# Gathered rows that change partition quarters through memory, with one gather a tile, in the expert stage of an attention and expert-layer kernel

## The reference, cut to what matters

```
logits = x @ w_gate
expert_idx = np.argmax(logits, axis=1)
gate_w = softmax(logits)[np.arange(N), expert_idx]
for e in range(E):
    mask = expert_idx == e
    h = np.maximum(x[mask] @ w1[e], 0.0)
    out[mask] = gate_w[mask, None] * (h @ w2[e])
```

## Time and profile before

| what | value |
|---|---|
| time, median of 3 runs | 1517.04 us (1516.64 to 1517.5) |
| time of the profiled execution | 1513.94 us |
| its span, first to last instruction | 1512.2 us |
| TensorE busy | 1466.0 us |
| VectorE / ScalarE / GpSimd busy | 913.9 / 633.1 / 616.8 us |
| mean granted TensorE clock | 0.989 of full speed |
| attention and first layer | to about 1008 us |
| expert stage | from there to the end |

### The profile page before, as it was taken

The page is one execution under the profiler, slowest core; times in us unless marked ns, Lnnn a source line. Parts: engine busy times, 40 slices in busy tenths (PEclk is TensorE's granted clock), DMA queues, the critical chain, the costliest instruction groups (busy, mean ns, idle before and its releaser), DMA issues.

```text
span 1512.2 us, 29278 instructions
## 1 busy us (share of the span) xinstructions
PE 1466.0 (97%) x7918; PEld 1264.5 (84%) x7919; DVE 913.9 (60%) x1669; ACT 633.1 (42%) x1291; POOL 616.8 (41%) x725
## 2 busy tenths in 40 slices
PE   7999999999999999999999999989899999999997
PEld 6999999999978888888888888877687778778885
DVE  4688888888825374655637465535466656665442
ACT  5688788788812223122222312223243434333221
POOL 5666676676710022020202202110554456666551
PEclk9999999999999999999999999999899999999999
DMA  7354444344430202020120202144677777764441
GB/s 253 114 140 103 108 107 106 102 108 127 107 122 0 70 15 83 0 83 28 56 69 14 83 0 83 15 137 140 191 215 224 232 219 225 226 209 152 143 144 51
DMA packets 113738, 174.05 MB, mean 115 GB/s; under 512 B 54960, under 2 KB 74672, under 8 KB 109474
## 3 DMA queue, kind: packets, MB, share of 16 engines
q1 hardware_dynamic: 104386, 153.39, 34.1%
q0 software_dynamic: 9312, 20.15, 4.3%
HBM read 123.64 MB, written 50.32 MB: 115 GB/s over the span
## 4 chain that ended last, share of the span: by engine, by line
PE 49%; DMA 11%; SPq 4%; issue 4%; POOL 2%; DVE 1%; ACT 1%; POOLq 0%; DVEq 0%; ACTq 0%
PE bank L173 48%; DMA h_scratch<-arena 5%; DMA arena<-we 2%; SPq L1019 1%; DMA rows_scratch<-arena 1%; POOL arena L1103 1%; DMA out<-arena,ids 1%; DMA arena<-rows_scratch,idgq 1%; SPq L830 1%; SPq L1039 1%; SPq L996 0%; DVE xturn L1478 0%; ACT arena L1228 0%; POOLq L830 0%; ACT big L816 0%
## 5 line engine op out<-in xcount | busy, mean ns | idle before, releaser
L173 PE MATMUL bank<-big,xs 128*128 (+1 forms) x2100 | 492.9, 395 | 22.0 <-DVE xs L1483 8.9
L173 PEld LDWEIGHTS bank<-big,xs 128*128 128x128 f32 x2100 | 398.4, 191 | 111.6 <-issue 29.2
L173 PE MATMUL bank<-xs,big 128*128 128x512 f32 x1728 | 397.5, 391 | 2.7 <-PEq L222 2.7
L173 PEld LDWEIGHTS bank<-xs,big 128*128 128x128 f32 x1728 | 324.7, 188 | 70.4 <-issue 3.0
L173 PE MATMUL bank<-big 128*128 128x512 f32 (+1 forms) x1632 | 328.4, 350 | 2.0 <-POOL big L312 1.4
L173 PEld LDWEIGHTS bank<-big 128*128 128x128 f32 (+1 forms) x1632 | 257.8, 166 | 36.7 <-POOL big L312 1.6
L1055 POOL TENSOR_TENSOR arena<-arena 128x512 f32<-128x512 f32 x32 | 46.8, 1473 | 433.3 <-DMA arena<-rec_scratch 433.3
L1440 DVE TENSOR_TENSOR arena<-arena,bank 128x512 f32<-128x512 f32 x72 | 49.4, 687 | 245.9 <-PE bank L173 245.9
L1103 POOL DMA_INDIRECT arena<-rows_scratch,idgq x144 | 146.2, 1015 | 65.9 <-issue 35.5
L1365 DVE CUSTOM_DVE_ANT_0 arena<-arena 128x512 f32<-128x512 f32 x256 | 159.3, 687 | 17.8 <-ACT arena L1220 17.8
L1198 ACT COPY arena<-bank 128x512 f32<-128x512 f32 x72 | 42.4, 589 | 287.9 <-PE bank L173 287.9
(11 more groups left out here) (186 smaller groups left out, 1351.0 us busy)
## 6 DMA issues: line engine op xcount, KB each, us to landing
arena<-we SPq DMA_DIRECT2D x32, 1024.0 KB, 6.0
h_scratch<-arena SPq DMA_DIRECT2D x37, 512.0 KB
arena<-h_scratch SPq DMA_DIRECT2D x148, 128.0 KB
kqraw<-kq SPq DMA_DIRECT2D x32, 576.0 KB, 3.8
xT_scratch<-arena SPq DMA_DIRECT2D x32, 288.0 KB
rows_scratch<-arena SPq DMA_DIRECT2D x36, 256.0 KB, 2.2
arena<-v SPq DMA_DIRECT2D x64, 128.0 KB, 2.4
arena<-xT_scratch SPq DMA_DIRECT2D x8, 1024.0 KB, 5.5
```

What stands on the lines that cost most here:

```text
L173: ins = nc.tensor.matmul(out, left[a], right[b], start=first and n == 0, stop=last and n == 2)
```

## The change

- One gather a tile of whole rows (`gather_far`), for tile g + 3 in place of g + 2. It waits until the rows before it in `xg` have been stored (`x_stored`), not until they have been transposed.
- SP stores `xg` to a scratch of 256 KB (`store_gathered`) and loads it back with quarters exchanged into a new buffer `xq` by four loads of 64 KB (`load_row_quarters`), once the store has landed and `turn_rows` has read `xq`. `turn_rows` reads `xq`.
- In the loop SP's order becomes: store and loads of tile g + 2's rows, store of tile g's hidden rows, weights, loads of the hidden rows. The semaphore `way_open` is only counted up, between waits.
- `idq`, its 16 loads, ScalarE's scaling and the list of quarters are gone. One more table entry is made on VectorE.
- In stage 2 the wait for the row stores, with the freeing of x2, moves from the end of a turn into the next one: ahead of the x loads, and in the last turn behind the loads of weights 0 and 1.
- Chunk 4 of the weights is loaded inside the last turn, ahead of its row stores, and chunk 5 ahead of the wait for these stores. Before, both came behind that wait.

```diff
@@ -131,7 +131,7 @@
-                        ("idq", NQ * E * TPE, F32), ("quarter", 1, U32), ("idgq", NQ, U32),
+                        ("cden", H * S // DK, F32), ("idfar", 1, U32), ("xq", DM, F32),

@@ -139,10 +139,8 @@
-    m["cden"] = m["idq"][:, 0:H * S // DK]
-    m["idf"] = arena[:, SLOTS * CW + 2 * FF:SLOTS * CW + 2 * FF + E * TPE].bitcast(U32)

@@ -158,6 +156,7 @@
+    m["xrows"] = nc.dram_tensor("x_scratch", [P, DM], F32).ap()

@@ -597,8 +596,6 @@
-            for a in range(NQ):
-                dve.memset(m["quarter"][a * (P // NQ):(a + 1) * (P // NQ), :], a)

@@ -852,7 +849,7 @@
-        idf_set, idq_in, xq_in = sem("s3_idf_set"), sem("s3_idq_in"), sem("s3_xq_in")
+        x_stored, xq_in, way_open = sem("s3_x_stored"), sem("s3_xq_in"), sem("s3_way_open")

@@ -956,8 +953,22 @@
             def load_weights(c):
                 sp.dma_start(m["stage"][:, (c % 2) * CW:(c % 2 + 1) * CW], t["we"][c]).then_inc(w_in[c % 2], 16)
+            def load(c):
+                slot = (c % SLOTS) * CW if isinstance(c, int) else sp.snap((c % SLOTS) * CW)
+                sp.wait_ge(w_here, 16 * c)
+                sp.dma_start(ahead[:, ds(slot, CW)], t["we"][ds(c, 1)].rearrange("a p n -> p (a n)")
+                             ).then_inc(w_here, 16)
+
+            def rows_landed(i):
+                if has_before(i):
+                    sp.wait_ge(rows_out, 16 * BQ * i)
+                    sp.sem_inc(x2_free, 1)
+
+            sp.sem_inc(w_here, 16 * CPE)
+
             def turn(i, more):
                 if more:
+                    rows_landed(i)
                     sp.wait_ge(x_lo, DC * i + DC)
                     load_x(sp, m, i + 1)
                     for c in range(DC):
@@ -971,17 +982,18 @@
                     load_weights(0)
                     load_weights(1)
+                    rows_landed(i)
                     for c in range(2, CPE):
                         sp.wait_ge(w_lo, c - 1)
                         load_weights(c)
+                    sp.wait_ge(lg_mm, BQ)
+                    sp.wait_ge(ab_lo, FC * NB)
+                    load(CPE)
                 for q in range(BQ):
                     sp.wait_ge(x2_gated, BQ * i + q + 1)
                     sp.dma_start(m["rows"][ds(i * BT + q * P, P), :], x2[:, q]).then_inc(rows_out, 16)
                 if not has_before(i):
                     sp.wait_ge(m["rec_out"], 16 * B + 16)
-                if more:
-                    sp.wait_ge(rows_out, 16 * BQ * i + 16 * BQ)
-                    sp.sem_inc(x2_free, 1)
             for u in range(2):
                 sp.wait_ge(m["nd_out"][u], 32 * PAIRS // 2)
@@ -990,12 +1002,6 @@
             load_den(sp, m, B - 1)
             turns(sp, turn)
-            def load(c):
-                slot = (c % SLOTS) * CW if isinstance(c, int) else sp.snap((c % SLOTS) * CW)
-                sp.wait_ge(w_here, 16 * c)
-                sp.dma_start(ahead[:, ds(slot, CW)], t["we"][ds(c, 1)].rearrange("a p n -> p (a n)")
-                             ).then_inc(w_here, 16)
-
             def load_into_slot_of(c):
                 sp.wait_ge(w_lo, c + 1)
                 load(c + SLOTS)
@@ -1019,32 +1025,53 @@
                     sp.dma_start(hq[a * Q:(a + 1) * Q, :].rearrange("i (b c) -> i b c", b=P // Q), stored[a]
                                  ).then_inc(hq_in, 16)
+            def store_gathered(g):
+
+                sp.wait_ge(gathered, 16 * g + 16)
+                sp.sem_inc(way_open, 1)
+                sp.wait_ge(xq_in, 16 * NQ * g)
+                sp.sem_inc(way_open, 1)
+                sp.dma_start(m["xrows"], xg).then_inc(x_stored, 16)
+
+            def load_row_quarters(g):
+
+                sp.wait_ge(x_stored, 16 * g + 16)
+                sp.sem_inc(way_open, 1)
+                sp.wait_ge(x_turned, g)
+                sp.sem_inc(way_open, 1)
+                stored = m["xrows"].rearrange("(b i) (a n) -> a i b n", i=Q, a=NQ)
+                for a in range(NQ):
+                    sp.dma_start(m["xq"][a * Q:(a + 1) * Q, :].rearrange("i (b n) -> i b n", b=P // Q), stored[a]
+                                 ).then_inc(xq_in, 16)
+
             def tile(g):
+                store_gathered(g + 2)
+                load_row_quarters(g + 2)
                 store_rows(g, hs)
+                loads_of(g - 1)
                 load_quarters(g)
-                loads_of(g - 1)
-
-            sp.sem_inc(w_here, 16 * CPE)
+
             sp.sem_inc(h_stored, 32)
             sp.sem_inc(hq_in, 128)
-            sp.wait_ge(lg_mm, BQ)
-            sp.wait_ge(ab_lo, FC * NB)
+            sp.sem_inc(x_stored, 16 * (FIRST + 1))
+            sp.sem_inc(xq_in, 16 * NQ * (FIRST + 1))
+            load(CPE + 1)
             sp.wait_ge(rows_out, 16 * BQ * NB)
-            for c in range(CPE, CPE + 3):
-                load(c)
-            sp.wait_ge(idf_set, 1)
-            idq = m["idq"][:].bitcast(U32).rearrange("p (b n) -> p b n", b=NQ)
-            for a in range(NQ):
-                for b in range(NQ):
-                    sp.dma_start(idq[a * Q:(a + 1) * Q, b], m["idf"][b * Q:(b + 1) * Q, :]).then_inc(idq_in, 16)
+            load(CPE + 2)
             sp.wait_ge(w_lo, CPE)
             sp.wait_ge(idt_mm, 1)
             sp.wait_ge(tabs, 2)
+            store_gathered(FIRST + 1)
             store_rows(2, hq)
+            load_row_quarters(FIRST + 1)
             load_quarters(2)
             load(CPE + 3)
-            tiles(sp, tile)
-            loads_of(last_of(sp, 1))
+            tiles(sp, tile, 2)
+            last1 = last_of(sp, 1)
+            store_rows(last1, hs)
+            load_quarters(last1)
+            loads_of(last_of(sp, 2))
+            loads_of(last1)
         @block.gpsimd
         def _(pool):
@@ -1087,24 +1114,18 @@
                 pool.indirect_dma_start(xg, None, m["rows"], bass.IndirectOffsetOnAxis(m["idg"][:, 0:1], 0)
                                         ).then_inc(gathered, 16)
-            def gather_quarters(g):
-
-                row = table(m, pool, ROW, g, 0, E * TPE - 1)
+            def gather_far(g):
+
+                row = table(m, pool, ROW, g, 0, E * TPE)
                 if isinstance(g, int):
-                    pool.wait_ge(xtr_mm, g)
-                else:
-                    pool.wait_ge(x_turned, g)
+                    pool.wait_ge(xtr_mm, FIRST + 1)
+                pool.wait_ge(x_stored, 16 * g)
                 pool.sem_inc(turn_taken, 1)
-                pool.tensor_tensor(m["idgq"][:], idq[:, :, ds(row, 1)].rearrange("p b n -> p (b n)"),
-                                   m["quarter"][:, 0:1].to_broadcast([P, NQ]), ALU.add).then_inc(idg_set, 1)
+                pool.tensor_copy(m["idfar"][:], m["idall"][:, ds(row, 1)]).then_inc(idg_set, 1)
                 pool.wait_ge(idg_set, g + 1)
                 pool.sem_inc(turn_taken, 1)
-                for b in range(NQ):
-                    pool.indirect_dma_start(xg[:, b * P:(b + 1) * P], None,
-                                            m["rows"].rearrange("r (a n) -> (r a) n", a=NQ),
-                                            bass.IndirectOffsetOnAxis(m["idgq"][:, b:b + 1], 0)).then_inc(xq_in, 16)
-
-            idq = m["idq"][:].bitcast(U32).rearrange("p (b n) -> p b n", b=NQ)
+                pool.indirect_dma_start(xg, None, m["rows"],
+                                        bass.IndirectOffsetOnAxis(m["idfar"][:, 0:1], 0)).then_inc(gathered, 16)
             def scatter(g):
                 pool.wait_ge(scattered, 16 * g)
@@ -1145,18 +1166,19 @@
             pool.sem_inc(idg_set, FIRST)
             gather(FIRST)
-            pool.wait_ge(idq_in, 16 * NQ * NQ)
-            gather_quarters(FIRST + 1)
+            gather_far(FIRST + 1)
             pool.wait_ge(y_sb, 2)
             pool.indirect_dma_start(t["out"], bass.IndirectOffsetOnAxis(m["ids0"][:, 0:1], 0), ysb, None,
                                     bounds_check=N - 1, oob_is_err=False).then_inc(scattered, 16)
+            gather_far(FIRST + 2)
             pool.wait_ge(tabs, 2)
             def period(g):
-                gather_quarters(g + 2)
+                gather_far(g + 3)
                 scatter(g - 2)
-            last = tiles(pool, period, 2)
+            last = tiles(pool, period, 3)
+            scatter(last_of(pool, 4))
             scatter(last_of(pool, 3))
             scatter(last_of(pool, 2))
             row = table(m, pool, ROW, last, 0, E * TPE)
@@ -1310,8 +1332,6 @@
             relu(1)
             rows_high(2)
-            act.wait_ge(idt_sb, 1)
-            act.mul(m["idf"], last_ps[:, 0:E * TPE], float(NQ)).then_inc(idf_set, 1)
             weights(CPE)
             relu_stored(2)
@@ -1473,10 +1493,10 @@
             def turn_rows(g):
-                dve.wait_ge(xq_in, 16 * NQ * g - 16 * NQ * FIRST)
+                dve.wait_ge(xq_in, 16 * NQ * g + 16 * NQ)
                 dve.wait_ge(h_mm, 2 * g)
                 dve.transpose(m["xturn"].rearrange("p (c b j) -> p c b j", c=DC, b=P // Q),
```

(3 more changed lines are left out.)

## The result

The changed kernel takes 1577.11 us (median of 4 runs) where the kernel before takes 1516.84 on the same chip: a ratio of 1.039 (1.037 to 1.042), 60 us slower. The forecast was slower too, but by 11 us, and its range ended at 1547. The profiled execution of the changed kernel took 1578.93 us, against 1513.94 before: 65 us between the two traces.

A forecast was written before the change was run, and what follows sets the result against it. TensorE, busy 97% of the span, was taken as the bound, SP's queue next. Gains ahead of the loop would be eaten by 12.6 us turns: second product 25 begins 11.5 us later, 1513.94 becomes 1525.4, median 1528 us; range 1497 to 1547.

The forecast's parts named there:

- x2's gap: Before x2's transposes, ahead of the loop: earlier weights 0 and 1 remove 4.9 us of gap and 3.4 of clock, 8.3 us.
- the prediction's own sign: Ahead of the loop: if TensorE's gap at 1003 stays, the step that removes it by earlier weights fails.
- the rival that named this: Ahead of the loop: moved waits do nothing, row stores and id scatters still hold weights; up to 8 us more, chance 0.05.
- Gather 3's gap: Before gather 3's transposes, ahead of the loop: gather 3 meets an idle queue, 2.3 + 1.7 = 4.0 us go.
- Start of the loop: Tile 4: gather 4 issued at about 1048.4, its hidden rows' store at 1084.3 where it stands near 1091 before.
- The turn: SP's loop turn with a weight load: 12.6 us a tile (12.2 to 13.5), against TensorE's 10.9 and 11.67 before.
- hidden store to weights: SP's loop turn: 0.39 us of issue and 1.94 us of table loads and branches, 2.33 us.
- weights' issue to the store's landing: SP's loop turn: weights, hidden rows and gathered rows' store pass one queue in order; 7.6 us (7.2 to 8.5).
- landing to hidden store: SP's loop turn: 0.3 us of waits, 2.1 for four row loads, 0.25 to the store, 2.65 us.
- Transfers do not hold each other: Loop: gathered rows' store takes its lone 2.2 us even behind weights, turn 10.4; 1490.6 us, or 1482; chance 0.12.
- The queue packs better: Loop: each DMA engine passes on after its own share of weights, 6.5 us for 7.6, turn 11.5; 1504 us; chance 0.18.
- The gather is late: Loop: SP waits for gather g+2, held on POOL behind a scatter waiting for y_sb; about 1550 us; chance 0.08.

The follow-up runs named there:

- 5: The changed kernel with weights 0 and 1 issued ahead of the second-last turn's row stores and id scatters; 1563.3 us, ratio 1.037 to the kernel before.
- 9: The kernel before with the change's stage 2 edits, and weights 0 and 1 issued ahead of the row stores and id scatters; 1499.2 us, ratio 0.993.
- 1: The changed kernel with the gathered rows' store issued a turn earlier, ahead of the weights; 1547.6 us, ratio 1.025 to the kernel before.
- 2: The changed kernel with the weights issued behind the loads of hidden rows; 1615.4 us, ratio 1.070 to the kernel before.
- The stage-2 part alone: The kernel before with only the moved row-store wait and the early loads of weights 4 and 5, loop untouched; 1504.7 us, ratio 0.997.
- 16: The changed kernel with the loop's 24 weight loads cut to their first eighth, all issues, waits and table reads kept; 1505.6 us, ratio 0.996.
- after: The changed kernel itself, against the kernel before; 1577.1 us, ratio 1.039.
- 7: The changed kernel with the gathered rows' store ahead of the weights and two scratch slots for those rows; 1532.0 us, ratio 1.016 to the kernel before.
- 10: The changed kernel with the early gathered store, two scratch slots, and hidden quarters' loads ahead of the weights; 1530.3 us, ratio 1.013 to the kernel before.
- 14: The changed kernel with the loop's weight loads issued by ScalarE on its own queue; 1583.9 us, ratio 1.050 to the kernel before.

## Why the prediction was right in direction and wrong in size

**Ahead of the loop, x2's gap: the step that failed outright.** It said the weights, issued earlier, would land by 997 to 998 behind the row stores. They landed at 1002.2 and 1005.2, 25 and 27 us after issue. The row stores and GpSimd's scatters of ids were issued in the same microseconds; in the trace the row stores landed at 997.1, the last scatter at 1002.4. The weights' packets ran from 987.5 to 1004.9 beside them and took 849 ns each on average, where the kernel before shows 371 for the same packets sent later. The gap at 1003 stayed (7.0 us and its stretch at half clock): by the prediction's own sign the first step fails. It bounded the landing by the earlier trace rows alone. Runs 5 and 9 show what was missing, a place ahead of the stores: there the gap is gone. The price of the rival that named this (up to 8 us) was right; its 0.05 was not.

**Gather 3's gap** went, as said, in every trace with the change or its stage-2 part. In runs 1 and 2 one of 1.8 and 0.6 us came instead ahead of the transposes of an earlier gather (`ids`, tiles 0 to 2). The stage-2 part alone gave 5 us where 8.3 + 4.0 were counted on; run 9, with the first gap gone, gave 0.7%, 11 us.

**Start of the loop.** Tile 4's hidden store was forecast at 1084.3 and came at 1096.65: 12.4 us late. Its gather was issued at 1056.7 instead of 1048.4, x2's 8.3 us not having gone, and took 5 us beside a scatter; the store was issued at 1061.89.

**The turn.** Forecast 12.6 (12.2 to 13.5), measured 14.3. From tile 4's hidden store to tile 25's it took 302.7 us (1096.65 to 1399.37) instead of 267.5: 35.2 us over 21 turns, the largest term. With the 12.4 above that is the 47.6 us by which tile 25's store missed its forecast of 1351.8; behind it the changed kernel took 177.8 us to its end where the forecast has 171.9. By the turn's three steps:
- hidden store to weights: 2.33 forecast, 3.22 measured. In the records of SyncE's instructions the second of the two table reads took 1.15 us instead of 0.27. In each such turn it lies beside the packets of GpSimd's gather; the two reads of 0.27 that the forecast was read off had the hidden rows' 1 KB pieces beside them. Run 16 has the same 3.1, so the weights' packets aren't its cause; that the gather's are is not shown.
- weights' issue to the store's landing: 7.6 forecast, 8.7 measured, above the high end of 8.5. The form of the sum was right (run 16: take the packets away and 2.9 of it goes). By the DMA records (medians of the turns with one load) the weights' last packet ends 4.9 us after their issue, as forecast, and the gathered store's 0.8 behind the hidden rows', as forecast. The hidden rows' last one ends 2.4 behind the weights', not 1.5 to 1.6: that term was read off the store of these 512 KB, and what stands there is their load in 512 pieces of 1 KB. And from the store's last packet to the row loads pass another 0.6, for which the sum had no term.
- landing to hidden store: 2.65 forecast, 2.4 measured.

So the loop's mechanism was right, and the terms of its sum that failed are the first step (0.9 us a turn too small), the load of the hidden rows (0.9) and the unpriced 0.6. Against them stand 0.4, by which the 7.6 lies above the low end, and the 0.3 of the last step: 1.7 us a turn in all.

Turns without weights measured 11.0, not 10.1 to 10.4: no longer covered by 10.9.

**The rivals.** "Transfers do not hold each other" (0.12) is refuted by 16 against after: 2.4 us alone, 5.3 behind weights. The 2.6 us estimate that stands with it is near the lone store's 2.1 and far from the 4.6 to 5.9 of the turns with weights. The fit in the Trainium skill ("DMA: Bandwidth & Descriptors", anatomy of one DMA) that it is worked out from is one for DMAs issued by GpSimd, and this store is issued by SyncE. "The queue packs better" (0.18) is refuted by the 8.7. "The gather is late" is refuted by SyncE's single wait at L1030. All three of the faster and even cases rested on a turn of 12.2 us or less, and the largest doubt was on the other side: every term was read from the kernel before, where the pieces it priced had not yet run beside each other.

**What stays open.** Why the gap before x2's transposes varies from 2.1 to 7.0 us with the same order of issues; why the table read is slow in the changed kernel; and whether larger pieces for the quarter loads would shorten the turn, which wasn't tried. Runs 1, 2, 7, 10 and 14 together bear out that the ring is held by whatever follows the weights on the DMA engines; the landing of each single transfer under another's packets is read from their times, and was not isolated one by one.

## What to carry to other kernels

A bulk load is free only as long as nobody in a closed ring of waits has to land behind it. When a change adds a store and a reload to such a ring, price the ring with the bulk load's packets in series at its worst place (here 2.7 us for 1 MB, against 0.5 before), and don't count on another order or another engine's queue to hide them: the eight orders, slots and queues tried here left the turn between 12.1 and 15.8 us. Shrinking the bulk load to an eighth, with every issue and wait kept, was the run that told how much of the ring it is; it should be the first.

Moving a wait doesn't move a landing: what counts is which transfers are ahead on the engines at the new place.

## What was not expected of the hardware

- With a load on ScalarE's queue a store on SyncE's lands about as late as with one in the same queue: 5.0 us after its issue in the median of the changed kernel's turns with weights, 4.9 in the median of run 14 (up to 6.8), 2.1 alone. In the turn of 14 that is shown, the store stood behind the hidden quarters of its own queue, and these behind the weights of the other: their first packet came 3.1 us after the issue, in the kernel before 1.0. The Trainium skill ("DMA: Bandwidth & Descriptors", queues, rings and completion order) says that an SDMA engine takes turns between the queue rows it has work for. That trace agrees in so far as both queues' packets share the engines; it shows that order within one DMA ring isn't needed for the delay.
- Two 1 MB loads issued behind four row stores and beside scatters of 4-byte ids took 24.65 and 27.25 us to land; 1 MB in the loop takes 5.4 (median).
- A register read from a table (`tab`) on SyncE took 0.27 us, with 1 KB pieces in flight too, and 1.1 to 1.2 us for the second read of each of the changed kernel's turns, beside the packets of GpSimd's gather.
